# A fused attention and two-MLP kernel: loads of q and k ahead of v, one copy moved, a projection half moved

## The reference

```python
def phi(x):
    proj = np.einsum('bhsd,df->bhsf', x, w_phi)
    proj = proj - np.max(np.abs(proj), axis=-1, keepdims=True)
    return np.concatenate([np.exp(proj), np.exp(-proj)], axis=-1)
q_p, k_p = (phi(q), phi(k))
kv = np.einsum('bhsf,bhsd->bhfd', k_p, v)
z = np.sum(k_p, axis=2)
num = np.einsum('bhsf,bhfd->bhsd', q_p, kv)
den = np.einsum('bhsf,bhf->bhs', q_p, z)[..., None] + 1e-06
attn = num / den
...
X = np.fft.fft(np.fft.fft(x, axis=1), axis=2)
u = x + np.real(X)
un = layernorm(u)
x = u + np.maximum(un @ w_ch1, 0.0) @ w_ch2
...
return x + np.maximum(layernorm(x) * g_ln @ w_ch1, 0.0) @ w_ch2
```

## Time and profile before

| what | value |
|---|---|
| median of 3 runs | 1019.16 us (1019.1 to 1019.36) |
| profiled execution | 1019.89 us, its span 1017.9 us |
| PE busy | 1007.9 us, 99% of the span |
| PEld, DVE, ACT, POOL busy | 934.7, 655.5, 591.6, 368.8 us |
| PE's share of the chain that ended last | 94% |

### The profile page before, as it was taken

One profiled execution on the slowest core, in us unless ns is written; L12 is line 12 of the kernel. 1 busy time (PEld: TensorE's weight loads), 2 busy tenths in 40 slices (PEclk: granted clock), 3 DMA queues, 4 the chain that ended last, 5 costly groups with the idle time before them and its releaser, 6 DMA issues.

```text
span 1017.9 us, 17119 instructions
## 1 busy us (share of the span) xinstructions
PE 1007.9 (99%) x6028; PEld 934.7 (92%) x6028; DVE 655.5 (64%) x1156; ACT 591.6 (58%) x1036; POOL 368.8 (36%) x364
## 2 busy tenths in 40 slices
PE   8999999999999999999999999999999999999998
PEld 8999999999998999999999999989989999999997
DVE  5576777788975658556585556756568455674443
ACT  6666576586565555555556566566665566644341
POOL 5622443345054325134442244341363332721210
PEclk9999999999999999999999999999999999999999
DMA  6233122220252322332232322323315323232102
GB/s 158 60 91 91 36 71 53 55 48 12 69 144 79 94 73 68 100 85 71 74 91 76 104 67 75 98 62 94 100 46 156 86 71 102 63 124 84 62 1 62
DMA packets 101314, 80.32 MB, mean 79 GB/s; under 512 B 56944, under 2 KB 81776, under 8 KB 101232
## 3 DMA queue, kind: packets, MB, share of 16 engines
q1 hardware_dynamic: 100992, 78.91, 28.0%
q10 hardware_dynamic: 240, 0.33, 0.1%
HBM read 66.10 MB, written 4.72 MB: 70 GB/s over the span
## 4 chain that ended last, share of the span: by engine, by line
PE 94%; ACT 2%; DMA 1%; SPq 1%; DVE 1%; issue 1%; POOL 0%; DVEq 0%; ACTq 0%; POOLq 0%
PE bank L1186 38%; PE bank L1163 34%; PE bank L407 6%; PE bank L420 4%; PE bank L365 3%; PE bank L390 3%; PE bank L661 2%; PE bank L681 2%; DMA rawqk<-qkT 1%; PE bank L359 1%; PE bank L425 1%; SPq L571 0%; SPq L581 0%; ACT qk_hi L442 0%; DVE xall L548 0%
## 5 line engine op out<-in xcount | busy, mean ns | idle before, releaser
L1186 PE MATMUL bank<-w2op,hid 128*128 128x512 f32 x1728 | 423.2, 390 | 0.0
L1186 PEld LDWEIGHTS bank<-w2op,hid 128*128 128x128 f32 x1728 | 321.6, 188 | 53.4 <-issue 0.3
L1163 PE MATMUL bank<-x_T,w1op 128*128 128x384 f32 x1152 | 208.0, 335 | 0.0
L1163 PEld LDWEIGHTS bank<-x_T,w1op 128*128 128x128 f32 x1152 | 201.1, 188 | 3.9
L1163 PE MATMUL bank<-x_B,w1op 128*128 128x384 f32 x864 | 173.5, 336 | 0.0
L1163 PEld LDWEIGHTS bank<-x_B,w1op 128*128 128x128 f32 x864 | 154.4, 188 | 11.4
L1358 POOL TENSOR_TENSOR w_sums<-st_w 128x256 f32<-128x256 f32 x48 | 49.5, 1031 | 225.0 <-DVE w1op L1394 225.0
L1474 DVE SCALAR_TENSOR_TENSOR hid<-part_s,hid 128x384 fp32r<-128x384 f32 x141 | 98.1, 722 | 37.7 <-ACT hid L1470 37.6
L1326 POOL TENSOR_TENSOR x_sums<-xraw 128x256 f32<-128x256 f32 x30 | 22.3, 765 | 194.4 <-ACT xraw L1278 124.3
L1415 DVE TENSOR_TENSOR w2op<-st_w,w2op 128x1024 fp32r<-128x1024 f32 x48 | 62.7, 1307 | 45.9 <-ACT w2op L1411 45.9
L1470 ACT ACTIVATE hid<-part_s 128x384 fp32r<-128x384 f32 x141 | 73.3, 524 | 31.1 <-DVE part_s L1444 31.1
(11 more groups left out here) (181 smaller groups left out, 1613.9 us busy)
## 6 DMA issues: line engine op xcount, KB each, us to landing
st_w<-w1a SPq DMA_DIRECT2D x24, 512.0 KB, 3.5
st_w<-w2a SPq DMA_DIRECT2D x24, 512.0 KB, 3.8
st_w<-w1b SPq DMA_DIRECT2D x24, 512.0 KB, 3.5
st_w<-w2b SPq DMA_DIRECT2D x24, 512.0 KB, 3.7
v<-v SPq DMA_DIRECT2D x16, 256.0 KB, 3.2
out<-xall SPq DMA_DIRECT2D x16, 256.0 KB, 2.1
rawqk<-qkT SPq DMA_DIRECT2D x14, 288.0 KB, 4.1
rawqk<-qkT SPq DMA_DIRECT2D x14, 256.0 KB, 3.7
```

The source lines that it names most:

```text
L1163: last = nc.tensor.matmul(dst, w1op[g % 2][:, a, W1OP.index(w), c, :], xop[x][:, b, c, :], start=name in ("M2", "M1", "M7") and k_ == 0, s ...
L1186: last = nc.tensor.matmul(acc[t0 + t][:, :], hid[name, g % 2][:, x, P * t:P * (t + 1)], w2op[g % 2][:, y, j, :], start=first and k_ == 0, ...
```

## The change

Four things are edited. SyncE's list of loads is put in the order qk(3), v(1), qk(4), v(2) and so on. In slots 2 to 13 unit 3, the first half of k, is issued directly in front of unit 4 instead of between two parts of `pe_kv`. In slots 6 and 10 S1 is issued behind unit 4, ahead of the first numerators, instead of behind them. In slot 15 ScalarE's copy of round 1 stands ahead of the extra rows and the copy of Q1.

```diff
@@ def pe_slot(pe, g)
         pe_kv(pe, l, 1)
-        pe_unit(pe, g, 3)
+        if g >= XT_SLOT:
+            pe_unit(pe, g, 3)
...
         pe_transpose(pe, l, 4)
+        if g < XT_SLOT:
+            pe_unit(pe, g, 3)
         pe_unit(pe, g, 4)
...
-        if a_ is not None and a_[1] == 0:
+        second = a_ is not None and a_[1] == 1
+        if a_ is not None and not second:
             pe_stepA(pe, a_[0], "S0")
+        if second and g < XT_SLOT:
+            pe_stepA(pe, a_[0], "S1")
...
         pe_num(pe, l, 0)
-        if a_ is not None:
-            pe_stepA(pe, a_[0], ("C0", "S1")[a_[1]])
+        if a_ is not None and not second:
+            pe_stepA(pe, a_[0], "C0")
+        if second and g == XT_SLOT:
+            pe_stepA(pe, a_[0], "S1")
@@ def act_slot(act, g)
             act_q_copy(act, b_, 0)
+        act_q_copy_out(act, l, 1)
+        if g == PAIRS - 1:
             act_exrow(act, *f_)
             act_q_copy(act, b_, 1)
-        act_q_copy_out(act, l, 1)
@@ SyncE's list
             for g in range(1, PAIRS):
-                if 1 < g < PAIRS - 1:
-                    sp_qk(sp, g + 1)
+                if g < PAIRS - 2:
+                    sp_qk(sp, g + 2)
                 sp_v(sp, g)
```

## The result

The changed kernel takes 1016.09 us (median of 8 runs, 1015.9 to 1016.57) against 1019.39 us before (8 runs, 1019.1 to 1019.84): a ratio of 0.9969, 95% interval 0.996 to 0.9978, so 3.30 us faster. Measured once more beside another version it took 1016.11 us against 1019.65. The forecast was 1016.0.

A forecast was written before the change was run, and what follows sets the result against it. TensorE, busy 1007.9 of 1017.9 us, was taken to bound the kernel. Gains of 1.90, 0.91 and 0.60 less 0.30 make 3.11 us, so 1019.16 - 3.11 = 1016.05, forecast 1016.0 us, range 1014.9 to 1017.2.

The forecast's parts named there:

- What bounds the kernel: TensorE, busy 1007.9 of 1017.9 us; gains only from its 10 us of waits or from matmuls starting closer together.
- the sum: All slots together: 1.90 + 0.91 + 0.60 - 0.30 = 3.11 us gained.
- Loads, 1.90: Slots 2, 3 and 10: earlier q and k loads remove TensorE's waits for ScalarE's copy, 0.86 + 0.55 + 0.49 us.
- v behind q and k, cost 0: SyncE's queue: v, now issued after q and k, still lands before pe_kv needs it, even in slot 2; nothing lost.
- Slot 15, 0.91: Slot 15: round 1's copy runs while the extra rows wait for VectorE, so TensorE's whole 0.91 us wait goes.
- Unit 3's neighbours, 0.60: TensorE, 12 slots: one change from pe_kv to a unit fewer in each, 0.05 us apiece, 0.60 us gained.
- VectorE's cover, cost 0: VectorE: k's first maximum starts later but fits in 1.96 us of idle time; exponentials keep 2.19 us cover.
- Slot 13, -0.30: Slot 13: TensorE arrives earlier and waits for a copy behind the layer norm's root; 0.30 us lost, between 0 and 0.75.
- S1, 0: Slots 6 and 10: moving S1 gains nothing, as the end of CX, awaited by the next division, does not move.
- The slower rival: Next slot's pe_kv waits for k's exponentials once delayed past 2.19 us cover, paid twelve times; above 1021.2 us; chance 4%.

The follow-up runs named there:

- S1 alone: Kernel before with only S1 moved, in slots 6 and 10, behind unit 4 and ahead of the first numerators: 1019.48 us against 1019.51.
- the copy alone: Kernel before with only ScalarE's copy of round 1 in slot 15 moved ahead of the extra rows and Q1's copy: 1018.74 us against 1019.51.
- loads alone: Kernel before with only SyncE's list of loads in the new order: 1017.68 us against 1019.51.
- the kernel with k's units late: Changed kernel with units 3 and 4 both behind the first numerators in slots 2 to 13: 1061.21 us in one run, against 1019.48 before.

## Why the prediction was right

**What bounds the kernel.** Right. The waits named were the ones that could go in the edited places, and nothing behind slot 16 gave the gain back: from the first MLP matmul to the last the traces of before and after agree to 0.01 us (751.46 us; the other traces lie within 0.05 of it).

**Slots.** What the prediction and the earlier trace rows call slot 4, from 72 to 80 us, is slot 5 (the `v` issued at 78.42 is that of pair 5), and the `pe_kv` at 86.08 is slot 6's. SyncE issues v of pair 1 and q and k of pair 3 in slot 1. No term of the sum changes by it.

**Loads, 1.90.** The mechanism was right and the whole was right to 0.1: alone they gave 1.83. What the sum missed is that the terms overlap. Slots 3 and 10, 1.04 of the 1.90, are also cured by moving unit 3. The total did not suffer, since each wait was counted once; the attribution did. Also, 1.90 is the wait of one execution: with the loads in their old order and unit 3 in its old place (S1 alone and the copy alone), slot 3 was 0.23 and 0.17 shorter and slot 10 0.04 and 0.47.

**v behind q and k, cost 0.** Right in the change. v landed in 2.9 us at the median and 3.9 at most, no later than ahead of q and k. Once the bytes ahead of v were doubled it landed in 4.0 us at the median. The Trainium skill's page "DMA: Bandwidth & Descriptors", section "Issuing engines are not separate DMA queues", says that DMAs run on the same 16 engines and interleave, whichever engine started them. The 4.0 us agree with that, but a v that simply stood in line behind q and k would be slower too, and no run here tells the two apart.

**Slot 15, 0.91.** Measured 0.92, with no wait in its place. ScalarE's timeline of slot 15 shows the copy in the idle time of the earlier trace rows:

```profile
233.07 0.58 ACT L519 COPY qfT<-bank 128x512 f32<-128x512 f32 x1 [0.78 <-PE bank L390]
233.69 0.72 ACT L698 ACTIVATE xall<-xall 1x256 f32<-1x256 f32 x2
```

**Unit 3's neighbours, 0.60.** Mechanism right, size a little small. In slots 7, 8, 11 and 12 it is 0.05 to 0.07, in slots 4, 5, 6 and 9 it is 0.06 to 0.12; the change less loads alone gives 0.79 over slots 2 to 12. Why it is more in some slots stays open. In the changed kernel unit 3 runs into unit 4 at 0.12 a matmul, and the `pe_kv` block ahead of round 4 takes 75.53 - 74.24 = 1.29:

```profile
74.24 1.45 PE L407 MATMUL bank<-v,feat_k 128*128 128x65 f32 x12
75.53 0.39 PE L390 MATMUL bank<-ident,feat_q 128*128 128x128 f32 x2
75.67 0.37 PE L365 MATMUL bank<-wbd_hi,qk_hi 128*128 128x256 f32 x1
```

**VectorE's cover, cost 0.** Right. Both maxima of k now run together, 1.39 us from 76.66, where the second stood alone, and in slot 5 the exponentials start 8.89 us behind the first `pe_kv` matmul (79.67 less 70.78) where they started 8.98 behind it (81.67 less 72.69):

```profile
76.66 1.39 DVE L474 TENSOR_REDUCE amax_k<-bank 128x4 f32<-128x512 f32 x2 [3.84 <-PE bank L365]
```

**Slot 13, -0.30.** Right against the kernel before: the slot is 0.28 longer, which with the neighbours' 0.05 makes 0.33, and the wait is for the copy behind the root, as forecast. But the slot is 0.43 longer than with the unit in its old place. The new wait is 0.47 (203.65 less 201.89, less the normal 1.29). The prediction did not see the wait of 0.11 that stood there already, without a bracket, and that goes when the unit is moved in the other slots alone; that what is left over fits the 0.30 so well is in part luck.

**S1, 0.** Right, alone and within the change.

**The slower rival** was the weakest step. It had the exponentials' cover of 2.19 us as the point from which a delay costs. With the exponentials 2.9 to 3.6 us later the kernel lost some 45 us; the formula, 12 slots at the delay less 2.19, gives 9 to 17. The copy of round 0, the banks and the Fourier splits give way before the exponentials do, and then the clock falls. The forecast did not rest on it, for the change itself did not make the exponentials later.

**Where the rest went.** The sum had 3.11, the medians 3.30 and 3.54, and the interval of the ratio allows 2.2 to 4.1 us, so by the times alone there is nothing to explain. The table has 3.76, 0.65 more than the sum: 0.28 in slots 2, 3 and 10, whose waits were taken a little too short; 0.20 more than 0.05 a slot for the neighbours; and 0.18 in slots 1 and 14, which is spread between profiles and no gain. The terms are confirmed slot by slot; that the medians fall within 0.1 us of the forecast 1016.0 is closer than terms with such a spread can promise.

## What to carry to other kernels

Read where a load is issued and which wait stands in front of it in its queue: here v's wait held up q and k, which did not need it, and the cure cost one exchanged pair of lines. An order of instructions can move such a wait too, so terms read from separate waits may be one cause; test each edit alone and the whole without it. Do not take the nearest consumer's slack as the cover of a delayed result: what stands behind it in the same engine's queue can have less, as the copies and the splits had here.

## What was not expected of the hardware

In the kernel with k's units late the granted clock fell five times to 0.50, that is to 1.2 of 2.4 GHz. Each fall came while TensorE stood idle; the idle times ended at 107.34 (2.58 us), 127.52 (1.57), 151.97 (2.23), 209.42 (1.57) and 233.89 (2.23). But the length of the idle time does not tell whether the clock falls. One of 1.33 us (ended at 76.63) left it at 1.00, and so did the longest of all, 2.60 us, which ended at 190.23 (the last row is a window, with the columns as above):

```profile
107.34 0.40 PE L661 MATMUL bank<-cs_hi,ee 128*2 128x290 f32 x1 [2.58 <-DVE ts_lo L783]
...
151.97 1.31 PE L407 MATMUL bank<-v,feat_k 128*128 128x130 f32 x5 [2.23 <-DVE xall L548]
...
190.23 0.29 PE L661 MATMUL bank<-cs_hi,ee 128*2 128x290 f32 x1 [2.60 <-DVE ts_lo L783]
...
168.44:209.38 40.94, 35.98 (x310) 34.78 (x309) 27.65 (x75) 22.53 (x38) 9.97 (x8) 1.00 0.20 44
```

The same wait at the same place of the program, for `ts_lo` at L661, once cost the clock and once did not; what decides it stays open. What it costs is plain: behind the wait of 2.23 us the stretch from 151.37 to 168.42 ran at 0.50, though TensorE was busy for 15.99 of its 17.05 us, some 8.5 us lost, about four times the wait.

Two traces of one program agree to 0.01 us in each slot from 2 on. Slots with nothing edited agree nearly as well in traces of different kernels (to 0.03 us against the profile of before, slot 14 apart), but not where TensorE waits behind a load of q and k: slot 10's wait was 0.49 us in one profile of unedited slots and absent in another.
